# In the overflow tile of a routed MoE stage, rows are held on TensorE while w1 streams; a gate's split moves to GpSimd

## The chip, the cores and the metric

One core of a Trainium2 chip runs the whole program as one launch. The metric is the device time of one execution in microseconds; the number quoted for a kernel is the median of its runs. The engines named below are TensorE (PE, with its weight loads shown apart as PEld), VectorE (DVE), ScalarE (ACT), GpSimd (POOL) and SyncE (SP).

## What is computed

Sparse attention gives 3072 rows of 512 values. Two mixture-of-experts layers with eight experts each follow. In the first one a row with a positive skip score goes to the expert of its largest gate logit, in the second one each expert takes exactly 384 rows, given out greedily by logit. The first layer is what the change is about:

```python
def _moe_ref(x, w_skip, w_gate, w1, w2):
    do_compute = x @ w_skip > 0
    xc = x[do_compute]
    logits = xc @ w_gate
    e_idx = np.argmax(logits, axis=1)
    ...                                   # gate_w: softmax value of the chosen expert
    for e in range(E):
        mask = e_idx == e
        h = np.maximum(xc[mask] @ w1[e], 0.0)
        y[mask] = gate_w[mask, None] * (h @ w2[e])
    out[do_compute] = xc + y
```

Then `_moe2_ref` takes `logits = x @ w_gate` over the new rows (the "second gate"), sorts all of them, assigns rows under the cap of 384 for each expert, and computes `relu(x @ w1[e]) @ w2[e]`.

## The kernel before, in words

**Precision.** Every large product is made of three: each float32 operand is split into a rounded high part and the rest, the low part (`xh`, `xl`, `w1h`, `w1l`, `hh`, `hl`, `w2h`, `w2l`). ACT makes a high part, DVE subtracts it from the source to make the low part, and TensorE multiplies high by high, high by low and low by high.

**Stages.** Attention comes first. The first MoE layer then runs over blocks k = 0 to 7, one for each expert, with up to 224 rows (a tile of 128 and one of 96, `WIDE1` = 224). An expert with more than 224 rows leaves the rest to overflow tiles of 128 rows; block E (= 8) is the first of these. A count `n` made on the chip says how many there are, and with this data there is one: the path `n > 0` and `n < 2` runs, and the loop `more(k)` for further tiles does not. A search for the thresholds of the second layer's assignment follows, and then the second layer over its eight experts.

**A block.** For block k TensorE first makes h, turned (1024 hidden values along partitions, rows along columns): `h_products(k, s, m)`, m = 0 to 7, each twelve matmuls that hold a 128x128 piece of w1 and stream `WIDE1` = 224 columns of x, in block E too, where only 128 columns are real. Bank `ph[m % 4]` receives them. ACT (`one_block`, L1309) writes relu(h) as `hh`, DVE (L1399) makes `hl`. ACT (L1312) and DVE (L1402) also split the eight pieces of w2. `y_products(k, t, c)`, c = 0 to 7 (L1159), holds the 128 rows' hidden values of piece c and streams 512 columns of w2 three times. DVE's `y_keep` (L1420) scales by the gate and adds x, POOL's `scatter` (L1012) stores the rows.

**The second gate.** Between the h groups of block k, `z_part(k - 1, ...)` makes the second gate's logits of block k - 1: TensorE turns its finished rows (L1115), four transposes at a time, ACT copies them (L1298), TensorE multiplies by the gate (L1125 with three bf16 parts of the gate for blocks 0 to 6, L1133 in float32 for block 7 and the overflow tile), DVE copies the result to `zo` (L1391, L1393), and POOL scatters it to a table in HBM (L1021). In which group of block k a part comes is said by `z_at(k)`: `Z_AT` = (1, 3, 4, 7) in general, `Z_LAST` = (2, 3, 4, 5) for block E. The three bf16 parts of the gate, `wg2_parts`, are made by `split_gate2()` on DVE (L1501 to L1504), as the first thing of `count_extra()`, which stands in `y_keep` of block 0 between its two tiles.

**The end of the layer.** When both scatters of block 7's logits have landed, POOL raises `z_all`, SP loads the whole table back (L980, `logits`), and DVE takes its limits (L1589 to L1591) after the `y_keep` of the overflow tile. TensorE turns the limits (L1231), runs two filler matmuls (L1207, `keep_busy`), makes the overflow tile's own logits (L1133) and places them (L1252); DVE opens the search (from L1624).

Each engine runs its own instruction list in the order of the code and waits on semaphores. On ACT, `next_parts(E, ...)` has split w1 and x of the overflow tile before `one_block(E)` starts.

## Time and profile before

| what | us |
|---|---|
| median of 3 runs | 798.75 (798.06 to 798.95) |
| profiled execution | 799.55 |
| its span, first to last instruction | 797.8 |
| last y matmul of block 7 to first y matmul of the overflow tile | 434.61 to 447.95 |
| last y matmul of the overflow tile | 453.20 |
| search opens on DVE | 458.47 |

The profile is of one execution, with its own time; the median is of others, 0.8 us shorter. In a row of the order of time the first number is the start in us from the span's start and the second the duration; a bracket at the end gives the idle time before it on its engine and what ended it. Matmuls overlap, so their durations add up to more than the time that they take; the pace is the distance from start to start.

### The profile page before, as it was taken

How to read it: one execution, taken by the hardware profiler on the slowest of the kernel's cores; microseconds unless marked ns; L12 is line 12 of the kernel's file. 1: busy time of each engine (PE TensorE's matmuls, PEld its weight loads, DVE VectorE, ACT ScalarE, POOL GpSimd, SP SyncE). 2: the span in 40 equal slices, each digit the busy share in tenths (PEclk: the TensorE clock that was granted, in tenths of full speed). 3: DMA queues.
4: the chain of work that ended last, by engine and by line, in shares of the span. 5: the costliest groups of instructions: out<-in, count | busy, mean ns of one | idle time of the engine just before them, and what ended most of it. 6: DMA issues, size and time to landing. Idle time of an engine off the chain costs nothing. (4 is left out here: it accounts for less than half of the span.)

```text
span 797.8 us, 15936 instructions
## 1 busy us (share of the span) xinstructions
PE 746.6 (94%) x5652; PEld 669.1 (84%) x5652; DVE 549.1 (69%) x1509; ACT 460.7 (58%) x935; POOL 164.5 (21%) x185
## 2 busy tenths in 40 slices
PE   2899999999959999999999929999999999999997
PEld 2899999999939888899888826888888888888895
DVE  6878778778378979787767567767676757585420
ACT  3889889899536554565555305554545363636360
POOL 8100000000030232222222102141424232323221
PEclk9999999999969999999999959999999999999999
DMA  8999999986265576645663016767767676759851
GB/s 179 219 217 243 233 210 237 203 236 152 104 202 174 191 245 231 213 148 180 230 236 124 17 54 221 189 212 189 220 186 221 184 222 184 223 170 309 231 120 44
DMA packets 64107, 151.66 MB, mean 190 GB/s; under 512 B 12294, under 2 KB 15750, under 8 KB 64016
## 3 DMA queue, kind: packets, MB, share of 16 engines
q1 hardware_dynamic: 52512, 114.77, 49.0%
q0 software_dynamic: 11504, 35.72, 18.0%
q8 instruction: 52, 0.85, 0.5%
q14 instruction: 39, 0.32, 0.1%
HBM read 118.84 MB, written 16.67 MB: 170 GB/s over the span
## 5 line engine op out<-in xcount | busy, mean ns | idle before, releaser
L1912 PE MATMUL r_ph<-r_xh,r_w1h 128*128 128x384 f32 x256 | 90.6, 354 | 0.3 <-ACT r_xh L2026 0.3
L1912 PE MATMUL r_ph<-r_xh,r_w1l 128*128 128x384 f32 x256 | 86.2, 337 | 0.0
L1912 PE MATMUL r_ph<-r_xl,r_w1h 128*128 128x384 f32 x256 | 85.8, 335 | 0.0
L599 ACT ACTIVATE pr<-pr,nmx 128x232 f32<-128x232 f32 (+1 forms) x192 | 79.9, 467 | 4.9 <-DVE nmx L705 3.5
L1149 PE MATMUL m_ph<-m_xh,m_w1h 128*128 128x224 f32 x288 | 80.5, 279 | 0.1
L1149 PE MATMUL m_ph<-m_xh,m_w1l 128*128 128x224 f32 x288 | 79.0, 274 | 0.0
L1149 PE MATMUL m_ph<-m_xl,m_w1h 128*128 128x224 f32 x288 | 79.0, 274 | 0.0
L705 DVE CUSTOM_DVE_ANT_0 pr<-sc,bias 128x232 f32<-128x232 f32 (+1 forms) x192 | 65.0, 375 | 19.1 <-PE sc L473 17.6
L606 ACT ACTIVATE prt<-tp 128x384 f32<-128x384 f32 (+1 forms) x128 | 65.4, 536 | 21.5 <-PE tp L485 18.0
L1926 PE MATMUL r_py<-r_w2h,r_hh 128*128 128x512 f32 x192 | 76.3, 397 | 0.0
L1926 PE MATMUL r_py<-r_w2h,r_hl 128*128 128x512 f32 x192 | 75.1, 391 | 0.0
L1926 PE MATMUL r_py<-r_w2l,r_hh 128*128 128x512 f32 x192 | 74.9, 390 | 0.0
L472 PE MATMUL sc<-kk,qh 128*128 128x256 f32 x192 | 59.2, 329 | 14.9 <-POOL shut L438 14.2
L513 PE MATMUL op<-vo,prt 128*128 128x128 f32 x384 | 69.8, 277 | 3.0 <-ACT prt L606 3.0
L1309 ACT ACTIVATE m_hh<-m_ph 128x224 fp32r<-128x224 f32 (+1 forms) x72 | 25.2, 350 | 82.0 <-PE m_ph L1149 80.8
L2030 ACT ACTIVATE r_hh<-r_ph 128x384 fp32r<-128x384 f32 x64 | 31.2, 488 | 61.1 <-PE r_ph L1912 61.1
L516 PE MATMUL op<-vp,prt 104*128 104x128 f32 x320 | 62.3, 276 | 0.0
L2016 ACT ACTIVATE r_w1h<-r_w 128x1024 fp32r<-128x1024 f32 x32 | 33.6, 1059 | 45.2 <-DMA r_w<-moe_w 45.1
L513 PEld LDWEIGHTS op<-vo,prt 128*128 128x128 f32 x384 | 55.9, 192 | 3.7 <-ACT prt L606 2.2
L1149 PEld LDWEIGHTS m_ph<-m_xh,m_w1h 128*128 128x128 f32 x288 | 55.3, 192 | 1.0 <-ACT m_xh L1276 0.6
L1149 PEld LDWEIGHTS m_ph<-m_xl,m_w1h 128*128 128x128 f32 x288 | 55.3, 192 | 0.3
L1149 PEld LDWEIGHTS m_ph<-m_xh,m_w1l 128*128 128x128 f32 x288 | 55.3, 192 | 0.0
(327 smaller groups left out, 1970.1 us busy)
## 6 DMA issues: line engine op xcount, KB each, us to landing
r_w<-moe_w SPq DMA_DIRECT2D x64, 512.0 KB, 5.1
m_w<-moe_w SPq DMA_DIRECT2D x36, 512.0 KB, 4.8
row_buf<-moe_w SPq DMA_DIRECT2D x9, 2048.0 KB, 8.4
r_w2l<-r_w POOLq DMA_DIRECT2D x32, 512.0 KB, 5.3
k_raw<-kI SPq DMA_DIRECT2D x64, 208.0 KB, 7.0
q_raw<-qT SPq DMA_DIRECT2D x64, 192.0 KB, 7.5
vo<-vL SPq DMA_DIRECT2D x16, 384.0 KB
x_rows<-row_buf SPq DMA_DIRECT2D x4, 1536.0 KB, 6.3
```

The source lines that it names most:

```text
L472: nc.tensor.matmul(to, qh[s][:, hh, q], kk[s][:, hh, keys], start=True, stop=False)
L513: last = nc.tensor.matmul(o, w[:, t * P:(t + 1) * P], v_own(s, hh, i), start=True, stop=(i == 0))
L516: last = nc.tensor.matmul(o, w[0:CA, c * P:(c + 1) * P], v_band(s, hh, i - 1), start=False, stop=True)
L599: nc.scalar.activation(pr[n % PRS][:, t, lo:CW], pr[n % PRS][:, t, lo:CW], ACT.Exp, bias=nmx[n % PRS][:, t:t + 1], scale=-1.0).then_inc(ex ...
L606: nc.scalar.activation(prt[item % PRTS][:, 0:w], tp[item % 2][:, 0:w], ACT.Copy).then_inc(kept, 1)
L705: v.tensor_tensor_reduce(out=pr[n % PRS][:, t, lo:CW], in0=src, in1=bias0[:, h, :] if tile0 else bias[:, h, :], scale=-SCALE, scalar=3e38, ...
L1149: last = nc.tensor.matmul(ph[m % 4][:, 0:WIDE1], w[:, c, m * P:(m + 1) * P], x[s][:, c, 0:WIDE1], start=(c == 0 and a == 0), stop=(c == KC ...
L1309: nc.scalar.activation(hh[:, m, 0:W], ph[m % 4][:, 0:W], ACT.Relu).then_inc(h_high, 1)
L1912: last = nc.tensor.matmul(ph[m % 4][:, 0:CAP], w[:, c, m * P:(m + 1) * P], x[:, c, :], start=(c == 0 and a == 0), stop=(c == KC - 1 and a ...
L1926: last = nc.tensor.matmul(py[g % 2][:], h[:, c, t * P:(t + 1) * P], w[:, c, :], start=(c == 0 and a == 0), stop=(c == FC - 1 and a == 2))
L2016: nc.scalar.activation(w1h[:, c, :], w1[:, c, :], ACT.Copy).then_inc(w1_high, 1)
L2030: nc.scalar.activation(hh[:, m, :], ph[m % 4][:, 0:CAP], ACT.Relu).then_inc(h_high, 1)
```

## The change

1. **`one_tile(k)` takes the place of `one_block(k, ...)`** for block E and for further overflow tiles, on TensorE, ACT and DVE. TensorE's `hidden(k, half, chunks)` holds the 128 rows (`x[0][:, c, 0:P]`, high or low) and streams 512 columns of w1: 2 halves of 4 chunks of 3 matmuls, 24 matmuls of 512 columns in place of 96 of 224. h then lies with rows along partitions in `ph[0]` and `ph[1]`. ACT keeps relu(h) in `hidden_rows` (the storage of `xg[1]`), two operations of 512 columns (`keep_hidden`); TensorE turns it, eight transposes into `ph[2]` and `ph[3]` (`turn_hidden`); ACT copies each half into `hh` (`high_part`) and DVE makes `hl` (`low_part`), 512 columns each. `y_products` stays, with its waits counted in halves.
2. **Order inside the tile.** The parts of the second gate for block 7 stand after chunks 0 and 1, after chunks 2 and 3, and between the two `turn_hidden`. `Z_LAST` is gone. ACT now waits at the start of the tile until block 7's rows are kept (`y_kept`), since `xg[1]` is overwritten.
3. **`split_gate2()`** leaves DVE's `count_extra()`; its four operations stand at the end of POOL's list for the attention stage, behind a wait for the tables' loads.

The core of the diff:

```diff
@@ POOL, end of the attention stage
+                pool.wait_ge(loaded, TABLE_LOADS * 16)
+                keep_link(g.tensor_copy(wg2_parts[:, :, 0, :], wg2[:]))
+                keep_link(g.tensor_tensor(wg2_rest[:], wg2[:], wg2_parts[:, :, 0, :], ALU.subtract))
+                keep_link(g.tensor_copy(wg2_parts[:, :, 1, :], wg2_rest[:]))
+                keep_link(g.tensor_tensor(wg2_parts[:, :, 2, :], wg2_rest[:], wg2_parts[:, :, 1, :], ALU.subtract))
@@ TensorE
+                def hidden(k, half, chunks):
+                    for c in chunks:
+                        if half == 0:
+                            for part in (x_high, x_low, w1_high, w1_low):
+                                pe.wait_ge(part, KC * k + c + 1)
+                        for a, (x, w) in enumerate(((xh, w1h), (xl, w1h), (xh, w1l))):
+                            last = nc.tensor.matmul(ph[half][:], x[0][:, c, 0:P], w[:, c, half * 4 * P:(half + 1) * 4 * P],
+                                                    start=(c == 0 and a == 0), stop=(c == KC - 1 and a == 2))
+                    if c == KC - 1:
+                        last.then_inc(h_done, 1)
+
+                def turn_hidden(k, half):
+                    pe.wait_ge(rows_kept, 2 * (k - E) + half + 1)
+                    for m in range(4):
+                        last = nc.tensor.transpose(ph[2 + half][:, m * P:(m + 1) * P], hidden_rows[:, (4 * half + m) * P:(4 * half + m + 1) * P], ident[:])
+                    last.then_inc(rows_turned, 1)
...
+                def one_tile(k):
+                    hidden(k, 0, (0, 1))
+                        z_part(k - 1, 1, 0)
+                    hidden(k, 0, (2, 3))
+                        z_part(k - 1, 1, 1)
+                    hidden(k, 1, range(KC))
+                    turn_hidden(k, 0)
+                        z_part(k - 1, 1, 3)
+                    turn_hidden(k, 1)
+                    pe.wait_ge(y_kept, tiles_before(k))
+                    for c in range(FC):
+                        y_products(k, 0, c)
@@ DVE
                 def count_extra():
-                    split_gate2()
                     z_rows_of_slots()
```

How the instructions stand in TensorE's list of the overflow tile before, from the second gate's multiplication (`m_pt<-wg,m_yt`) of block 7 to the y products (`m_py`); `m_ph` is h, turned:

```order
L1149 MATMUL m_ph<-m_xl,m_w1h 128x224
L1149 MATMUL m_ph<-m_xh,m_w1l 128x224
L1133 MATMUL m_pt<-wg,m_yt 128x8 x4
L1133 MATMUL m_pt<-wg,m_yt 96x8 x4
L1149 MATMUL m_ph<-m_xh,m_w1h 128x224
...
L1159 MATMUL m_py<-m_w2h,m_hh 128x512
```

The same place in TensorE's list of the changed kernel (`m_ph<-ident,m_xg` turns the relu rows, which lie in `xg[1]`):

```order
L1203 MATMUL m_ph<-m_w1h,m_xh 128x512
L1203 MATMUL m_ph<-m_w1h,m_xl 128x512
L1203 MATMUL m_ph<-m_w1l,m_xh 128x512
L1211 MATMUL m_ph<-ident,m_xg 128x128 x4
L1144 MATMUL m_pt<-wg,m_yt 128x8 x4
L1144 MATMUL m_pt<-wg,m_yt 96x8 x4
L1211 MATMUL m_ph<-ident,m_xg 128x128 x4
L1172 MATMUL m_py<-m_w2h,m_hh 128x512
```

Two groups of h (24 matmuls) stood behind the gate's multiplication; now all of h stands ahead of it, and four transposes stand on each side.

ACT's list of the changed kernel for the whole overflow tile (`m_w2h` are the pieces of w2, `m_yt` the turned rows of block 7, `m_xg<-m_ph` the relu, `m_hh<-m_ph` the copy of the turned half):

```order
L1370 ACTIVATE m_w2h<-row_buf 128x512 x2
L1346 ACTIVATE m_yt<-m_pt 128x224 x2
L1370 ACTIVATE m_w2h<-row_buf 128x512
L1374 ACTIVATE m_xg<-m_ph 128x512
L1370 ACTIVATE m_w2h<-row_buf 128x512
L1346 ACTIVATE m_yt<-m_pt 128x224 x2
L1370 ACTIVATE m_w2h<-row_buf 128x512
L1374 ACTIVATE m_xg<-m_ph 128x512
L1378 ACTIVATE m_hh<-m_ph 128x4x128
L1370 ACTIVATE m_w2h<-row_buf 128x512
L1378 ACTIVATE m_hh<-m_ph 128x4x128
L1370 ACTIVATE m_w2h<-row_buf 128x512 x2
```

Before, this list was eight pairs of `m_hh` (128x128) and `m_w2h`, with the two pairs of `m_yt` behind the third and the fourth; now five pieces of w2 stand ahead of the first `m_hh`.

DVE's list of the changed kernel from the first w2 pieces of the overflow tile (`m_zo` is the copy of block 7's logits):

```order
L1493 TENSOR_TENSOR m_w2l<-row_buf,m_w2h 128x512 x5
L1497 TENSOR_TENSOR m_hl<-m_ph,m_hh 128x4x128
L1474 COPY m_zo<-m_pt 128x8
L1474 COPY m_zo<-m_pt 96x8
L1493 TENSOR_TENSOR m_w2l<-row_buf,m_w2h 128x512
L1497 TENSOR_TENSOR m_hl<-m_ph,m_hh 128x4x128
L1493 TENSOR_TENSOR m_w2l<-row_buf,m_w2h 128x512 x2
```

Before, `m_zo` stood behind the sixth piece of w2 and six `m_hl` of 128 columns; now it stands behind the first half's `m_hl`.

## Rows read from the trace of the kernel before

**Rows 1.** The page's row of h, high times high

```profile
L1149 PE MATMUL m_ph<-m_xh,m_w1h 128*128 128x224 f32 x288 | 80.5, 279 | 0.1
```

**Rows 2.** Waits of TensorE, 264 to 462 us: total us, times, longest

```profile
PE m_pt L1115 <- DVE row_buf L1420: 0.2, 1, 0.2
PE m_ph L1231 <- DVEq L1592: 0.2, 1, 0.2
```

**Rows 3.** Order of time, TensorE, overflow tile: start, duration, line, operation

```profile
434.84 0.27 PE L1149 MATMUL m_ph<-m_xh,m_w1h 128*128 128x224 f32 x1
...
438.85 0.56 PE L1115 MATMUL m_pt<-ident,row_buf 128*128 128x128 f32 x4
...
443.70 1.64 PE L1133 MATMUL m_pt<-wg,m_yt 128*128 128x8 f32 x16
...
447.95 0.40 PE L1159 MATMUL m_py<-m_w2h,m_hh 128*128 128x512 f32 x1
...
453.20 0.40 PE L1159 MATMUL m_py<-m_w2h,m_hl 128*128 128x512 f32 x1
```

**Rows 4.** Order of time, TensorE, four transposes of 128 rows

```profile
483.99 0.66 PE L1898 MATMUL r_ph<-ident,r_xg 128*128 128x128 f32 x4
484.48 0.38 PE L1934 MATMUL r_py<-lane_grid,onesb 128*128 128x512 bf16 x1
```

**Rows 5.** Order of time, ACT, then DVE, overflow tile

```profile
437.71 0.28 ACT L1309 ACTIVATE m_hh<-m_ph 128x128 fp32r<-128x128 f32 x1 [0.49 <-PE m_ph L1149]
437.89 0.63 ACT L1312 ACTIVATE m_w2h<-row_buf 128x512 fp32r<-128x512 f32 x1
...
435.04 0.75 DVE L1420 SCALAR_TENSOR_TENSOR row_buf<-m_py,gates,m_xg 96x512 f32<-96x512 f32 x1 [3.10 <-PE m_py L1159]
...
438.02 0.29 DVE L1399 SCALAR_TENSOR_TENSOR m_hl<-m_ph,m_hh 128x128 fp32r<-128x128 f32 x1
438.54 0.69 DVE L1402 TENSOR_TENSOR m_w2l<-row_buf,m_w2h 128x512 fp32r<-128x512 f32 x1 [0.23 <-ACT m_w2h L1312]
```

**Rows 6.** The page's row of ACT's larger h

```profile
L2030 ACT ACTIVATE r_hh<-r_ph 128x384 fp32r<-128x384 f32 x64 | 31.2, 488 | 61.1 <-PE r_ph L1912 61.1
```

**Rows 7.** Order of time and DMA issues, block 7's logits (KB, us to landing)

```profile
445.38 0.23 DVE L1393 COPY m_zo<-m_pt 128x8 f32<-128x8 f32 x2
...
450.43 0.34 SPq L980 DMA_DIRECT2D logits<-gate_logits  x1
...
logits<-gate_logits SPq DMA_DIRECT2D x1, 96.0 KB, 2.0
```

**Rows 8.** Order of time, all engines, end of the layer

```profile
453.75 0.75 DVE L1420 SCALAR_TENSOR_TENSOR row_buf<-m_py,gates,m_xg 128x512 f32<-128x512 f32 x1 [3.02 <-PE m_py L1159]
...
454.41 0.34 DVE L1589 TENSOR_REDUCE m_limits<-logits 128x1 f32<-128x192 f32 x1
...
455.98 0.95 PE L1133 MATMUL m_pt<-wg,m_yt 128*128 128x8 f32 x8
```

**Rows 9.** Order of time, DVE and TensorE, end of block 0

```profile
261.28 0.17 DVE L1501 CAST wg_parts<-wg 128x32 bf16<-128x32 f32 x1
...
262.16 0.17 DVE L1434 TENSOR_SCALAR m_lanes<-m_pt 128x16 f32<-128x16 f32 x1
```

**Rows 10.** The page's row of DVE's costliest operation in attention

```profile
L705 DVE CUSTOM_DVE_ANT_0 pr<-sc,bias 128x232 f32<-128x232 f32 (+1 forms) x192 | 65.0, 375 | 19.1 <-PE sc L473 17.6
```

**Rows 11.** Waits from 26 to 236 us; order of time, POOL

```profile
POOL m_never L1024 <- POOLq L214: 201.6, 1, 201.6
...
18.68 0.34 POOL L446 CAST ids<-idsf 128x48 bf16<-128x48 f32 x1
```

**Rows 12.** Busy us by stretch (PE, PEld, DVE, ACT, POOL), granted clock

```profile
445.00:450.00 5.00, 5.00 (x38) 4.66 (x37) 2.84 (x10) 1.59 (x4) 2.35 (x2) 1.00 0.01 1
...
460.00:462.00 2.00, 0.00 (x0) 0.00 (x0) 1.21 (x7) 0.00 (x0) 0.00 (x0) 0.71 0.00 0
478.00:480.00 2.00, 2.00 (x15) 1.12 (x14) 1.00 (x4) 0.81 (x1) 0.00 (x0) 0.50 0.84 307
```

More of the change, by code:

```diff
@@ L897, in z_at, with hidden_before @@
             def z_at(k):
-                return () if not isinstance(k, int) or k == 0 else Z_LAST if k == E else Z_AT
+                return Z_AT if k else ()
+            def hidden_before(k):
+                return FC * k if isinstance(k, int) and k <= E else 2 * k + (FC - 2) * E
             def in_parts(k):
@@ L1154, in y_products @@
                     if t == 0:
-                        for part in (h_high, h_low, w2_high, w2_low):
+                        for part in (h_high, h_low):
+                            pe.wait_ge(part, FC * k + c + 1 if isinstance(k, int) and k < E else hidden_before(k) + c // 4 + 1)
+                        for part in (w2_high, w2_low):
                             pe.wait_ge(part, FC * k + c + 1)
@@ L1314, in one_block, with one_tile, w2_part, keep_hidden @@
                             z_part(k - 1, z_at(k).index(m))
+                def one_tile(k):
+                    act.wait_ge(y_done, tiles_before(k))
+                    act.wait_ge(y_kept, tiles_before(k))
+                    act.wait_ge(w2_loaded, 16 * k + 16)
+                    def w2_part(m):
+                        nc.scalar.activation(w2h[:, m, :], w2[:, m, :], ACT.Copy).then_inc(w2_high, 1)
+                    def keep_hidden(half):
+                        act.wait_ge(h_done, hidden_before(k) + half + 1)
+                        nc.scalar.activation(hidden_rows[:, half * 4 * P:(half + 1) * 4 * P], ph[half][:], ACT.Relu).then_inc(rows_kept, 1)
+                    def high_part(half):
+                        act.wait_ge(rows_turned, 2 * (k - E) + half + 1)
+                        nc.scalar.activation(hh[:, 4 * half:4 * half + 4, 0:P], ph[2 + half][:].rearrange("p (m n) -> p m n", n=P), ACT.Copy).then_inc(h_high, 1)
+                    w2_part(0)
+                    w2_part(1)
+                    if isinstance(k, int):
+                        z_part(k - 1, 0)
+                    w2_part(2)
+                    keep_hidden(0)
+                    w2_part(3)
+                    if isinstance(k, int):
+                        z_part(k - 1, 1)
+                    w2_part(4)
+                    keep_hidden(1)
+                    high_part(0)
+                    w2_part(5)
+                    high_part(1)
+                    w2_part(6)
+                    w2_part(7)
                 for s in range(2):
@@ L1336, in _ @@
                     next_parts(E, 0, P)
-                    one_block(E, P)
+                    one_tile(E)
                     for i in range(4):
@@ L1406, in one_block, with one_tile, w2_part, low_part @@
                             gates_of_slots()
+                def one_tile(k):
+                    def w2_part(m):
+                        dve.wait_ge(w2_high, FC * k + m + 1)
+                        v.tensor_tensor(w2l[:, m, :], w2[:, m, :], w2h[:, m, :].bitcast(F32), ALU.subtract).then_inc(w2_low, 1)
+                    def low_part(half):
+                        dve.wait_ge(h_high, hidden_before(k) + half + 1)
+                        v.tensor_tensor(hl[:, 4 * half:4 * half + 4, 0:P], ph[2 + half][:].rearrange("p (m n) -> p m n", n=P),
+                                        hh[:, 4 * half:4 * half + 4, 0:P].bitcast(F32), ALU.subtract).then_inc(h_low, 1)
+                    for m in range(5):
+                        w2_part(m)
+                    low_part(0)
+                    if isinstance(k, int):
+                        z_part(k - 1, 1, 3)
+                    w2_part(5)
+                    low_part(1)
+                    w2_part(6)
+                    w2_part(7)
                 def y_keep(k, s):
@@ L1645, in more @@
                     next_parts(k, 0, P)
-                    one_block(k, P)
+                    one_tile(k)
                     y_keep(k, 0)
@@ L1653, in _ @@
                 with dve.If(n > 1):
-                    one_block(E, P)
+                    one_tile(E)
                     y_keep(E, 0)
```

22 lines of the change are left out of this document (11 added, 11 removed).

## The prediction, made before the changed kernel was run

> **What bounds the kernel now.** I read the page's costliest groups first. One row of h in the first MoE layer has 288 matmuls [rows 1], 32 for each of nine blocks: eight experts and one overflow tile. So the overflow tile runs, and its h streams 224 columns like every other block's. The view of who waited for whom for TensorE, from the end of block 0 to the end of the layer, has only two rows, of 0.2 us each [rows 2]. In these 200 us TensorE is the bound: what is taken from its list shortens the layer, as long as nobody makes it wait. The view in order of time gives the tile [rows 3]: h starts at 434.84, the y products at 447.95, the last of these at 453.20. ACT and DVE have idle time between their pieces there [rows 5]. The rows at the end of the layer show a second chain beside the y products: block 7's logits are scattered, loaded back, and DVE's limits need them [rows 7, 8].
>
> **TensorE's share of the tile.** The 36 matmuls of 224 columns from 434.84 to 438.85 [rows 3] have a pace of 4.01 / 36 = 0.111 us. Removed: 96 x 0.111 = 10.7 us. Added: 24 matmuls of 512 columns. The y products have this very shape, 128 held columns and 512 streamed in float32 parts, and their 24 take (453.20 - 447.95) / 23 = 0.228 us each [rows 3], so 5.5 us. Added too: eight transposes of 128 rows. Four of them take 484.48 - 483.99 = 0.49 us [rows 4], so 1.0 us. The block 7 parts (two groups of four transposes and the sixteen narrow matmuls) are in both kernels and only change place. Sum: -10.7 + 5.5 + 1.0 = **-4.2 us**, y products from about 443.7 in place of 447.95. The bounds of a transposing group are the 0.49 us and nothing at all (the weight loads might hide them): gain 4.2 to 5.2.
>
> **Does the new chain hold TensorE up?** New is that h passes ACT, TensorE, ACT and DVE before the first y product. By the paces above, 24 matmuls and the two transposing groups of block 7 end at 434.84 + 5.5 + 0.84 = 441.16. The 0.84 is what rows 3 leave from 434.84 to 443.70 beside 72 matmuls of 0.111. The last matmul is done some 0.2 us later. ACT's relu of 512 columns out of PSUM isn't in this tile. From 0.28 us for 128 columns [rows 5] and 0.49 for 384 [rows 6] a line gives 0.59; four times the small one is 1.12, the upper end. ACT also needs the first half's copy (0.59), and DVE its low part: 0.69 us for 512 columns out of SBUF [rows 5], upper end four times 0.29 = 1.16. With my values: 441.4 + 0.6 + 0.6 + 0.7 = 443.3. TensorE meanwhile turns the first half (0.49), does the sixteen narrow matmuls (from 443.70 to 447.95 less 24 x 0.111, so 1.58) and turns the second half (0.49): 443.7. The chain is hidden with **0.4 us** to spare, and I take no wait, since the line through two measured sizes is nearer than four separate operations. With all upper ends it ends at 444.8, and TensorE waits 1.1 us. The second half is needed only by the fifth y chunk, twelve matmuls or 2.7 us later, and is ready about 445.2 against 446.5. The w2 pieces cost ACT 0.63 and DVE 0.69 each [rows 5]; the last is ready near 446.3 against a need at 448.5. ACT's new wait for block 7's kept rows ends at 435.8 (DVE's operation from 435.04, 0.75 us) [rows 5]; it holds the w2 pieces behind it, the first of which came behind a relu before, and so not ahead of the first twelve matmuls (434.84 + 12 x 0.111 = 436.2). It costs nothing.
>
> **Where the gain can be caught: the logits.** DVE copies block 7's logits at 445.38, SP loads the table at 450.43, and it lands 2.0 us later, 452.43 [rows 7]. The limits start at 454.41, right behind the kept y rows [rows 8], so this chain has 2.0 us of slack now. In the changed order the narrow matmuls start at 441.16 + 0.49 = 441.65 in place of 443.70 [rows 3], **2.05 us** earlier, against 4.2 for the y rows. DVE is free for the copy at 443.3, as it is due. So the table lands at 450.4 while the y rows would allow the limits at 450.2: the slack is used up, and 0.2 us of the gain goes to a new wait for a DMA. TensorE turns the limits and runs two fillers ahead of the tile's own logits, from 455.98 [rows 8], so this wait is passed on in full. Gain so far **4.0 us**; if landing counts from the end of the issue (0.34 us, rows 7), 3.7.
>
> **The gate's split.** On DVE its four operations take from 261.28 to 262.16 [rows 9], 0.88 us, ahead of the keep of block 0's second tile, for which TensorE waits 0.2 us [rows 2]. All but these 0.2 us were hidden; gain **0.2 us**, bounds 0 and 0.25. On GpSimd they stand where it sits idle for 201.6 us [rows 11]; a cast of 48 columns takes 0.34 us there, so four such are 1.4 us, hidden by that idle time. Nothing else is behind the new wait on GpSimd's list until the MoE layer. For DVE the bounds are no delay, and 1.4 us in attention if it were shut out for all of it; I take none, since DVE's own work there leaves it idle for 19.1 us, of which 17.6 are waits for TensorE [rows 10].
> The Trainium skill has a rule against this part ("SBUF — State Buffer", section "Who interferes with whom"): a DVE instruction with two SBUF inputs and a GpSimd instruction that reads SBUF shut each other out, the later one waits for the whole of the earlier. No row here shows such a block; by the rule DVE could lose up to those 1.4 us once, and the sum would be 2.8 in place of 4.2 if TensorE passed all of it on.
>
> **Sum.** 4.0 + 0.2 = 4.2 us. The profiled execution took 799.55 us, its span 797.8: after, 795.3 and 793.6. The median of the runs is 0.8 below that execution, so the predicted median is 798.75 - 4.2 = **794.5 us**. The search and the second layer follow the limits through dependences alone, so I let them shift as they are.
>
> **Rivals.**
> 1. *The relu chain ends last.* With the upper ends above, y starts 1.1 us late, and DVE's copy of the logits, which stands behind the first low part, comes at 444.8 in place of 443.3, so the table lands at 451.9. Gain 454.4 - 451.9 + 0.2 = 2.7: 796.05 us. For it: four PSUM passes in a row where there was one pair. Against: the two ACT sizes lie on a flat line.
> 2. *The logits decide by more.* If GpSimd's scatters or the load take 1 us longer from their earlier start, the limits wait 1.2 us: 795.5. For it: their slack is exactly used up. Against: they start into a stretch with no other transfer.
> 3. *Slower: the clock falls in the tile.* TensorE's granted clock is 1.00 from 445 to 450, with the narrow matmuls in it, and 0.50 (1.2 GHz) from 478 to 480 after the search's short bursts; it fell between 460 and 462, a stretch with no TensorE work in it [rows 12]. If it fell when the turning starts at 441.2, the 2.6 us up to the y products and their 5.5 us would take twice as long: +8.1, 802.6 us. From 4.2 us of work at 1.2 GHz on, the change no longer pays. Against: the stretch has no idle time by my sum, and the narrow matmuls and transposes of the kernel before left the clock at 1.00. The Trainium skill speaks for this one ("TensorE: Matmul & The Clock Gate", section "Part 4: PE-mode transpose"): transposes don't count as work for the clock in the way that matmuls do. By it eight more transposes bring the fall nearer; the row from 445 to 450 is against it here.
> 4. *The gain is given back later.* The search and the fillers ahead of the second layer come 4.2 us earlier. From 478 to 480 the clock was still at 0.50 [rows 12]. If it rises later against the fillers, TensorE enters the second layer at 1.2 GHz. To eat all of the gain this needs 4.2 us of work there at the full clock's price done at half: 798.7, no change. Against: TensorE was busy for all of those 2 us, so it works towards the rise well ahead of the layer.
>
> That the change doesn't do what it says is out: the tile's matmuls are in the trace, and the order of instructions shows theirs replaced.
>
> **Chances.** Forecast (793.6 to 795.4) 0.66; rival 1 0.12; rival 2 0.13; rival 3 0.04; rival 4 0.05. What a measurement of this kernel can tell from no change is about 0.2%, 1.6 us: faster means under 797.15, where the forecast and rivals 1 and 2 lie, and half of rival 4's partial cases, 0.92. Within 0.2%: 0.05. Slower: 0.03, the full form of rival 3. The range takes in rivals 1 and 2 and the unknown costs. Below: transposing groups at no cost bring the narrow matmuls, and the table, another 0.49 us forward (gain 4.7, 794.05), less 0.45 us, half of the spread of the three runs. Above: rival 1 and about as much: **793.6 to 796.6**.
>
> **What would show it.** Right: 24 matmuls of 512 columns at 0.228 us; y products starting about 443.5 with no idle TensorE ahead of them; the wait of 0.2 us at the end of block 0 gone and what follows 0.2 us earlier; a DVE idle time of some tenths ahead of the limits, ended by the load; the table load issued about 448.2. Wrong: idle TensorE ahead of the first y product, ended by DVE (rival 1); a wait of over 1 us ahead of the limits (rival 2); a granted clock under 1.00 between 440 and 450 (rival 3); the opening of the search 4.2 us earlier but the end less so (rival 4).

## The result, and the profile after

The changed kernel takes **794.01 us** (median of four runs, 793.26 to 794.20), beside 798.64 (also of four) for the kernel before. The ratio is 0.9936, 95% interval 0.9924 to 0.9949. Applied to the 798.75 us of the first table, that is a gain of 5.1 us, 4.1 to 6.1, or about 793.6 us; the two medians by themselves differ by 4.6 us. The prediction had a gain of 4.2 and a range from 793.6 up. The time by the ratio lies at that very edge, too near to call it inside or outside, and the interval of the gain holds the forecast. The prediction was right in sign and in the tile's mechanism; its gain was too small, and the bounds of one of its terms were wrong.

The profiled execution took 794.11 us with a span of 792.4 (before: 799.55 and 797.8), so 5.4 us less between first and last instruction. The mean granted clock was 0.975 in both.

TensorE in the overflow tile, in order of time, of the changed kernel (start, duration, line, operation, the idle time ahead of it and what ended it). It answers to [rows 3]:

```profile
434.15 0.39 PE L1203 MATMUL m_ph<-m_w1h,m_xh 128*128 128x512 f32 x1
...
438.88 0.39 PE L1203 MATMUL m_ph<-m_w1l,m_xh 128*128 128x512 f32 x1
...
440.24 0.39 PE L1203 MATMUL m_ph<-m_w1l,m_xh 128*128 128x512 f32 x1
440.47 0.60 PE L1211 MATMUL m_ph<-ident,m_xg 128*128 128x128 f32 x4
440.91 1.64 PE L1144 MATMUL m_pt<-wg,m_yt 128*128 128x8 f32 x16
442.40 0.64 PE L1211 MATMUL m_ph<-ident,m_xg 128*128 128x128 f32 x4
442.79 0.48 PE L1172 MATMUL m_py<-m_w2h,m_hh 128*128 128x512 f32 x1
...
448.12 0.40 PE L1172 MATMUL m_py<-m_w2h,m_hl 128*128 128x512 f32 x1
```

From 434.15 to the first y product are 8.64 us; before, from 434.84 to 447.95, 13.11. No row of TensorE's matmuls or weight loads there has idle time in a bracket, and the starts follow one another at the usual pace: the relu chain doesn't hold TensorE up. The seven matmuls from 438.88 to 440.24 lie 0.227 us apart, the pace that the y products had. The first turning group costs 440.91 - 440.47 = 0.44 us, the second 442.79 - 442.40 = 0.39.

ACT and DVE beside it, the relu chain and the copy of block 7's logits; it answers to [rows 5, 7]:

```profile
440.67 0.60 ACT L1374 ACTIVATE m_xg<-m_ph 128x512 f32<-128x512 f32 x1 [1.02 <-PE m_ph L1203]
441.16 0.59 ACT L1378 ACTIVATE m_hh<-m_ph 128x512 fp32r<-128x512 f32 x1
441.79 0.69 DVE L1497 TENSOR_TENSOR m_hl<-m_ph,m_hh 128x512 fp32r<-128x512 f32 x1 [1.41 <-ACT m_hh L1378]
442.58 0.23 DVE L1474 COPY m_zo<-m_pt 128x8 f32<-128x8 f32 x2
```

The row at 441.79 ends at 442.48, and the first y product starts at 442.79: 0.3 us between them. Not all of it is slack, as e5_relu_in_four_pieces shows below.

The end of the layer, all engines, in order of time; it answers to [rows 7, 8]:

```profile
443.68 0.99 POOL L1032 DMA_INDIRECT gate_logits<-m_zo,m_zrows  x1 [6.33 <-DVE m_zo L1474]
444.98 1.41 POOL L1032 DMA_INDIRECT gate_logits<-m_zo,m_zrows  x1 [0.30 <-issue]
447.66 0.34 SPq L991 DMA_DIRECT2D logits<-gate_logits  x1
448.65 0.75 DVE L1522 SCALAR_TENSOR_TENSOR row_buf<-m_py,gates,m_xg 128x512 f32<-128x512 f32 x1 [1.94 <-PE m_py L1172]
449.63 0.35 DVE L1683 TENSOR_REDUCE m_limits<-logits 128x1 f32<-128x192 f32 x1 [0.23 <-DMA logits<-gate_logits]
```

The limits now wait 0.23 us for the loaded table, right behind the kept rows. From start to start it costs a little more: they start 0.98 us behind the keep at 448.65, where in the kernel before it was 454.41 - 453.75 = 0.66 [rows 8], so 0.3 us.

Where the gain lies. The columns are distances between marks in order of time in each kernel's trace, in us. Block 0 runs from ACT's first `hh` to the turning of block 0's rows on TensorE; the tile from DVE's keep of block 7's last rows to the limits; the entry from the search's `best` (L1624 before) to the first `r_hh` of the second layer; the second layer from there to the end of the span.

| kernel | block 0 | blocks 1 to 7 | tile | entry | second layer |
|---|---|---|---|---|---|
| before | 25.88 | 167.77 | 19.37 | 33.44 | 305.90 |
| before, again | 25.88 | 167.87 | 19.37 | 33.04 | 305.98 |
| changed | 25.50 | 167.85 | 15.28 | 33.15 | 305.52 |
| changed, again | 25.48 | 167.85 | 15.28 | 32.90 | 305.52 |
| tile alone | 25.89 | 167.77 | 15.20 | 33.21 | 305.76 |
| split alone | 25.49 | 167.86 | 19.37 | 32.92 | 305.45 |

Before against changed: tile -4.09, block 0 -0.38, blocks 1 to 7 +0.08, entry -0.29, second layer -0.38. The rest of the 5.4 us, -0.39, lies ahead of block 0's first `hh`, 241.39 us from the span's start before and 241.00 changed. Five runs whose kernels are the same up to the tile (changed, again, e4, e5 and e9 below) reach this mark anywhere from 240.56 to 241.58, so I read nothing into it. The entry too differs by 0.2 to 0.4 between two executions of one kernel.

The second layer's column needs a cut of its own. From the last y product to the end of the span the two executions of the kernel before take 5.50 and 5.75 us, so the end of the program scatters by 0.25. From the first `r_hh` to the last y product they take 300.40 and 300.23, the changed kernel 300.06 and 300.03: about 0.2 to 0.4 us are gained on TensorE itself.

### The profile page after: what moved, and what is told of

Same layout as the page of the kernel before. It is cut to its first block and busy times, and to the rows that moved or that the text cites. A ratio compares the mean times of both kernels' runs of the same rounds, so it can differ in the third digit from the quotient of the medians.

```text
span 792.4 us, 15792 instructions
## 1 busy us (share of the span) xinstructions
PE 740.9 (94%) x5585; PEld 662.7 (84%) x5588; DVE 548.1 (69%) x1499; ACT 461.7 (58%) x931; POOL 165.9 (21%) x189
## 5 line engine op out<-in xcount | busy, mean ns | idle before, releaser
L1160 PE MATMUL m_ph<-m_xh,m_w1h 128*128 128x224 f32 x256 | 71.5, 279 | 0.1
L1160 PE MATMUL m_ph<-m_xl,m_w1h 128*128 128x224 f32 x256 | 70.2, 274 | 0.0
L1160 PE MATMUL m_ph<-m_xh,m_w1l 128*128 128x224 f32 x256 | 70.2, 274 | 0.0
L1357 ACT ACTIVATE m_hh<-m_ph 128x224 fp32r<-128x224 f32 x64 | 22.9, 358 | 69.0 <-PE m_ph L1160 69.0
L1172 PE MATMUL m_py<-m_w2h,m_hh 128*128 128x512 f32 (+1 forms) x136 | 55.3, 407 | 0.0
L490 PE MATMUL tp<-ident,pr 128*128 128x128 f32 x352 | 54.4, 273 | 0.2 <-ACT prt L611 0.2
L1172 PE MATMUL m_py<-m_w2l,m_hh 128*128 128x512 f32 (+1 forms) x136 | 53.3, 392 | 0.0
```

Of the source, the lines that this page charges most:

```text
L490: last = nc.tensor.transpose(tp[item % 2][:, c * P:(c + 1) * P], parts[c], ident[:])
L1160: last = nc.tensor.matmul(ph[m % 4][:, 0:WIDE1], w[:, c, m * P:(m + 1) * P], x[s][:, c, 0:WIDE1], start=(c == 0 and a == 0), stop=(c == KC ...
L1172: last = nc.tensor.matmul(py[t % 2][0:r, :], h[:, c, t * P:t * P + r], w[:, c, :], start=(c == 0 and a == 0), stop=(c == FC - 1 and a == 2))
```

## The experiments

**Theory.** The gain is the tile's 24 wide matmuls in place of 96 narrow ones, less two turning groups, with the table load catching 0.2 us; the split gives the stall at the end of block 0. **Rivals.** The gain of the tile comes from its 96 dead columns; the relu chain or the load is close to deciding; the clock can fall in this tile; and for the part that I had not foreseen, that VectorE's list, not the tile, changed the second layer.

### The two kernels again

> The kernel before, unchanged, as a second profile of it. The 5.4 us between the two profiled spans fall into 0.34 up to the MoE layer's first w1 parts, 0.35 at the end of block 0, 4.1 from there to the limits, 0.3 at the entry of the second layer and 0.35 within it. Theory (the first, fourth and fifth come from one execution, not from the kernel): this profile differs from the first one of the same kernel by some tenths of a us in these three stretches, either way, and the ratio to the kernel before is 1.000 within 0.001. Rival (the change shortens them too): they are within 0.1 us of the first profile.

The kernel before again: 799.12 us, ratio 0.9994 (0.9985 to 1.0003).

> The changed kernel as it is, timed in five rounds. My sum of 4.2 us gives a ratio of 0.9947; the tile and the split as the profile shows them, 4.1 + 0.35 = 4.45 us, give 0.9944; all of the 5.4 us of the two profiled spans would be 0.9932. Theory: 0.994 to 0.995. Rival (something outside the tile and block 0 gained another 0.9 us): 0.9932 or less.

The changed kernel again: 793.83 us, ratio 0.9937 (0.9924 to 0.9950). Both repeat, in time and in the table above: the marks of tile and block 0 to within 0.02 us. Of the stretches outside them the entry moved by some tenths between two executions, as e0's theory said, and the second layer didn't (0.08 us): its shortening isn't chance of one execution. e1's 0.9937 lies between its theory (0.994 to 0.995) and its rival (0.9932), and the interval holds both.

### One part at a time

> The tile's part alone: the gate is split on VectorE again, as before. Theory: the wait of TensorE at the end of block 0 is back at 0.2 to 0.35 us, first limits operation of the layer 4.1 us earlier than before relative to the tile's start; gain 4.0 to 4.1 us, ratio 0.9949. Rival (the split is worth more than its wait, since GpSimd's list or VectorE's backlog in block 1 matters): the gain falls to 3.5 us or less, ratio over 0.9955.

```diff
@@ the changed kernel, POOL
-                keep_link(g.tensor_copy(wg2_parts[:, :, 0, :], wg2[:]))
... (the wait and the other three operations too)
@@ DVE
                 def count_extra():
+                    split_gate2()
                     z_rows_of_slots()
```

Measured: 794.85 us, ratio 0.9955 (0.9941 to 0.9968), 3.6 us, between the theory's 4.0 and the rival's 3.5, and the interval holds both. The trace decides for the tile: 15.20, so 4.17 shorter, with block 0 at 25.89 as in the kernel before.

> The gate's split alone: four operations on GpSimd in attention, the tile as before. Theory: gain 0.2 to 0.35 us, ratio 0.9996 to 0.9998, which the times can hardly tell from none; in the trace TensorE's wait ahead of the transposes of block 0's rows is gone and block 1 is 0.2 to 0.35 us earlier relative to block 0's first h. Rival (GpSimd and VectorE shut each other out in attention): a VectorE operation with two SBUF inputs is longer than its 0.94 or 1.02 us beside the four operations, and attention ends up to 1 us later. The Trainium skill ("SBUF — State Buffer", "Who interferes with whom") would have the later one of the two wait.

```diff
@@ the kernel before, POOL, end of the attention stage
+                pool.wait_ge(loaded, TABLE_LOADS * 16)
+                keep_link(g.tensor_copy(wg2_parts[:, :, 0, :], wg2[:]))
+                ...
@@ DVE
                 def count_extra():
-                    split_gate2()
                     z_rows_of_slots()
```

Measured: 798.07 us, ratio 0.9987 (0.9979 to 0.9996), so 1.0 us, 0.3 to 1.7. Tile 19.37 as before, block 0 25.49, second layer 305.45. The two parts add up: 3.6 + 1.0 = 4.6, beside 5.1 measured together, within the intervals. All of the block 0 gain is the split's and all of the tile's gain the tile's. The split is worth more than the 0.2 us that I gave it: the trace shows 0.39 at block 0 alone.

Why block 0 gives 0.39 where the view of waits says 0.2. TensorE there, in order of time, of the kernel before:

```profile
266.75 0.27 PE L1149 MATMUL m_ph<-m_xh,m_w1l 128*128 128x224 f32 x1
267.27 0.61 PE L1115 MATMUL m_pt<-ident,row_buf 128*128 128x128 f32 x4 [0.25 <-DVE row_buf L1420]
```

and of the split alone:

```profile
266.56 0.28 PE L1154 MATMUL m_ph<-m_xh,m_w1l 128*128 128x224 f32 x1
266.67 0.55 PE L1120 MATMUL m_pt<-ident,row_buf 128*128 128x128 f32 x4
```

The idle time in the bracket is counted from the end of the last matmul, 267.02, and that end lies 0.27 us behind its start though the next one may start 0.11 behind it. From start to start the stall is 267.27 - 266.75 - 0.11 = 0.41 us, and with the split gone the distance is the plain pace of 0.11. The row of the weight load at the same place shows nearly all of it:

```profile
267.27 0.40 PEld L1115 LDWEIGHTS m_pt<-ident,row_buf 128*128 128x128 f32 x4 [0.43 <-DVE row_buf L1420]
```

The first three of GpSimd's four operations of the changed kernel, and DVE's operation beside the first, in order of time:

```profile
69.59 1.02 DVE L686 TENSOR_TENSOR kk<-k_raw,kk 64x832 fp32r<-64x832 f32 x1 [0.94 <-ACT kk L598]
```

```profile
69.77 0.91 POOL L455 CAST wg_parts<-wg 128x32 bf16<-128x32 f32 x1 [47.63 <-DMA step_t<-steps]
70.77 0.25 POOL L456 TENSOR_TENSOR wg_rest<-wg,wg_parts 128x32 f32<-128x32 f32 x1
71.08 0.21 POOL L457 CAST wg_parts<-wg_rest 128x32 bf16<-128x32 f32 x1
...
```

The first cast took 0.91 us and a cast of the same shape two rows on 0.21. The first began 0.18 us into DVE's operation with two SBUF inputs and ended just behind it (70.68 against 70.61); DVE's 1.02 us is what this operation takes elsewhere. That is the case of the Trainium skill ("SBUF — State Buffer", section "Who interferes with whom"), with the later one, here GpSimd, waiting for the earlier. It isn't that the first cast is slow behind a long idle time: in the changed kernel's second execution the first cast took 0.21 us and the second operation, which began 0.26 us into DVE's, 0.90; in the split alone none of the four met such an operation of DVE, and all took 0.21 to 0.25. Where DVE's operation began just behind a GpSimd cast it lost a little itself: 1.05 us in that second execution, 1.08 in e8. In the changed kernel's profile it lost nothing.

### The logits earlier, and the second turning between y chunks

> In the overflow tile block 7's logits come earlier: TensorE turns the first half of the relu rows and makes the logits after half of the second h half, turns the second half behind the first y chunk; ACT's and VectorE's lists follow. The same instructions in number. Theory (the table load now ends last ahead of the limits, by some 0.2 us): the logits' copy is 1.3 us earlier relative to the tile's start, the table load is issued about 1.3 us earlier, VectorE's wait for it ahead of the limits is gone, y products still without a wait, search opens 0.2 to 0.3 us earlier than in the changed kernel; ratio to before 0.9940 to 0.9945. Rival (the chain of relu rows ends last): TensorE waits ahead of the fifth y chunk or the first, and nothing is gained or some tenths are lost.

```diff
@@ TensorE, one_tile
-                    hidden(k, 1, range(KC))
+                    hidden(k, 1, (0, 1))
                     turn_hidden(k, 0)
                     if isinstance(k, int):
                         z_part(k - 1, 1, 3)
-                    turn_hidden(k, 1)
+                    hidden(k, 1, (2, 3))
                     pe.wait_ge(y_kept, tiles_before(k))
                     for c in range(FC):
                         y_products(k, 0, c)
+                        if c == 0:
+                            turn_hidden(k, 1)
```

ACT's and DVE's lists follow it: the first half's copy ahead of the fifth piece of w2, the second relu behind the sixth. Measured: 794.34 us, ratio 0.9939 (0.9926 to 0.9952), tile 15.28: nothing gained. The limits follow the kept rows without a wait, so the load's part was as I read it; but this is TensorE then, in order of time, with ACT's second relu:

```profile
443.18 0.60 ACT L1376 ACTIVATE m_xg<-m_ph 128x512 f32<-128x512 f32 x1 [1.32 <-PE m_ph L1203]
...
443.44 0.40 PE L1172 MATMUL m_py<-m_w2h,m_hl 128*128 128x512 f32 x1
...
443.83 0.66 PE L1211 MATMUL m_ph<-ident,m_xg 128*128 128x128 f32 x4
...
450.10 0.34 DVE L1686 TENSOR_REDUCE m_limits<-logits 128x1 f32<-128x192 f32 x1
```

The turning starts 0.39 us behind the last y product of chunk 0 where the pace is 0.23: it waits for the relu, which ends at 443.78. These 0.16 us are lost under the modelled end of a matmul, so the matmul's row has no bracket; the weight load beside it has one, of 0.42 us, ended by ACT's `m_xg`. With them and some more about the restart the keep of the tile's rows comes 0.30 us later than in the changed kernel, which takes the place of the 0.3 that the load had cost. So the first half of the theory held, and the rival named what was then in the way.

> The tile of e4_logits_earlier (block 7's narrow matmuls in the middle of the second half of h), with the second turning moved behind the second y chunk. Everything is computed. If the 0.16 us of wait ahead of that turning and what it cost to go on again are what ate the 0.2 us of the vanished wait for the table: no wait ahead of it, the limits 15.0 to 15.1 us after the keep of block 7's last rows in place of 15.28, 793.7 to 793.9 in all. If turning between y chunks costs more than turning ahead of them (the weight loads of a y chunk are not prepared behind a transpose): 15.3 or more, no gain over the changed kernel.

```diff
@@ the kernel of e4_logits_earlier
-                        if c == 0:
+                        if c == 1:
                             turn_hidden(k, 1)
```

Measured: 794.89 us, ratio 0.9941 (0.9926 to 0.9957), tile 15.40. The first expectation fell. The wait ahead of the turning is gone, but the one for the low part of the same half has come. TensorE and DVE, in order of time:

```profile
444.39 0.60 PE L1211 MATMUL m_ph<-ident,m_xg 128*128 128x128 f32 x4
444.75 0.48 PE L1172 MATMUL m_py<-m_w2h,m_hh 128*128 128x512 f32 x1
...
445.66 0.69 DVE L1499 TENSOR_TENSOR m_hl<-m_ph,m_hh 128x512 fp32r<-128x512 f32 x1 [0.61 <-ACT m_hh L1380]
...
445.99 0.40 PE L1172 MATMUL m_py<-m_w2h,m_hl 128*128 128x512 f32 x1
...
446.45 0.48 PE L1172 MATMUL m_py<-m_w2h,m_hh 128*128 128x512 f32 x1
```

The fifth chunk starts 0.46 us behind its forerunner, 0.23 late, and 0.1 behind the end of the low part (446.35). The time came out as its rival said (15.3 or more), but not for the rival's reason, that turning between y chunks costs more by itself: the turning took 444.75 - 444.39 = 0.36 us, less than in the changed kernel. None of the three orders beats another by more than 0.12 us; the tile is within some tenths of having every side chain end at the same time.

### The relu chain made longer

> The changed kernel with the relu, its copy and the low part done in four operations of 128 columns each instead of one of 512, in both halves. It prices rival 1 of the prediction: ends of 4 x 0.28 and 4 x 0.29 us. Theory: the chain gets 3 x 0.2 to 3 x 0.5 us longer (operations overlap by about 0.1 us each), VectorE's low part of the first half ends 0.5 to 1.4 us later, against 0.3 us of cover: TensorE waits 0.3 to 1.1 us ahead of the first y product, and the limits come 0.5 to 1.3 us later than in the changed kernel, since the logits' copy stands behind the low part. Rival (the chain has more cover than it seems, as TensorE's first y product is held by something else): no wait and the same time.

```diff
@@ the changed kernel, ACT (the copy to hh and DVE's low part likewise)
-                        nc.scalar.activation(hidden_rows[:, half * 4 * P:(half + 1) * 4 * P], ph[half][:], ACT.Relu).then_inc(rows_kept, 1)
+                        for m in range(4):
+                            last = nc.scalar.activation(hidden_rows[:, (half * 4 + m) * P:(half * 4 + m + 1) * P], ph[half][:, m * P:(m + 1) * P], ACT.Relu)
+                        last.then_inc(rows_kept, 1)
```

Measured: 793.99 us, ratio 0.9943 (0.9930 to 0.9956), the tile 15.64 in place of 15.28. ACT, DVE and TensorE, in order of time:

```profile
440.08 0.79 ACT L1375 ACTIVATE m_xg<-m_ph 128x128 f32<-128x128 f32 x4 [0.84 <-PE m_ph L1203]
...
440.73 0.82 ACT L1381 ACTIVATE m_hh<-m_ph 128x128 fp32r<-128x128 f32 x4
...
441.58 0.88 DVE L1502 TENSOR_TENSOR m_hl<-m_ph,m_hh 128x128 fp32r<-128x128 f32 x4 [1.62 <-ACT m_hh L1381]
...
442.67 0.47 PE L1172 MATMUL m_py<-m_w2h,m_hh 128*128 128x512 f32 x1 [0.23 <-issue]
```

Against the keep of block 7, DVE's low part ends 0.57 us later and the y products start 0.47 us later (8.91 for 8.44), the limits 0.36. So of the 0.3 us between the low part's end and the first y product only 0.1 was slack: even when TensorE waited, it started 0.21 us behind that end. The chain was hidden in the changed kernel, and it bounds the tile as soon as it grows by more than a tenth. Four operations of 128 columns take 0.79 us together, not the 4 x 0.28 that my rival 1 added up: behind one another they overlap.

### The dead columns, or the number of matmuls

> The kernel before, with w1 held as before, but the overflow tile streams only its 128 real columns in place of 224 in its 96 matmuls of h. No instruction added. Theory (what the tile pays for is the number of weight loads as much as the columns: a load of 128x128 takes 0.19 us in the rows): the pace falls from 0.111 to 0.06 to 0.10 us, and 96 of them gain 1 to 5 us; by columns alone it would be 0.111 x 128 / 224 = 0.063, gain 4.6 us, as much as the change itself. Rival (the weight load sets the pace already): 0.111 stays and nothing is gained. The Trainium skill ("TensorE: Matmul & The Clock Gate", Part 2) gives about 0.081 us for such pairs with 128 columns, which would be 2.9 us.

```diff
@@ the kernel before, TensorE, h_products
-                            last = nc.tensor.matmul(ph[m % 4][:, 0:WIDE1], w[:, c, m * P:(m + 1) * P], x[s][:, c, 0:WIDE1],
+                            W = width(k)
+                            last = nc.tensor.matmul(ph[m % 4][:, 0:W], w[:, c, m * P:(m + 1) * P], x[s][:, c, 0:W],
```

`width(k)` is 128 for the overflow tile: the old tile without its 96 dead columns. Measured: 801.75 us, ratio 1.0037 (1.0025 to 1.0049), **slower**. TensorE and its weight loads at the tile's start, and TensorE near its end, in order of time:

```profile
434.83 0.28 PE L1150 MATMUL m_ph<-m_xh,m_w1h 128*128 128x128 f32 x1
...
435.95 0.27 PE L1150 MATMUL m_ph<-m_xl,m_w1h 128*128 128x128 f32 x1
...
446.34 0.41 PE L1150 MATMUL m_ph<-m_xl,m_w1h 128*128 128x128 f32 x1
446.55 0.41 PE L1150 MATMUL m_ph<-m_xh,m_w1l 128*128 128x128 f32 x1
...
448.58 0.63 PE L1160 MATMUL m_py<-m_w2l,m_hh 128*128 128x512 f32 x1
449.01 0.63 PE L1160 MATMUL m_py<-m_w2h,m_hl 128*128 128x512 f32 x1
```

```profile
434.88 0.19 PEld L1150 LDWEIGHTS m_ph<-m_xl,m_w1h 128*128 128x128 f32 x1
```

Ten distances from 434.83 to 435.95 give 0.112 us a matmul, the same as with 224 columns. The theory's 0.06 to 0.10 and the page's 0.081 didn't come; the rival, that 0.111 stays, did. So the columns beyond 128 cost nothing in this stream: each matmul has a load of 128x128 held values, 0.19 us by its row and overlapping its neighbours, one for every 0.11 us (that it is the load that sets it is the nearest reading; no run changed the load alone). Here cutting columns from 224 to 128 saves nothing and cutting the number of matmuls does; the tile's gain is the second.

The other half of the result, which no expectation had, is the clock. The view by stretch (PE, PEld, DVE, ACT and POOL busy, then the granted clock, DMA share, GB/s):

```profile
...
446.00:447.00 1.00, 1.00 (x9) 1.00 (x8) 0.37 (x2) 0.80 (x2) 0.80 (x1) 0.67 0.00 0
447.00:453.00 6.00, 6.00 (x18) 4.94 (x18) 2.51 (x8) 0.80 (x2) 1.31 (x1) 0.50 0.07 18
453.00:454.00 1.00, 1.00 (x6) 0.82 (x5) 0.00 (x0) 0.00 (x0) 0.00 (x0) 0.92 0.00 0
```

From 446.3 to about 453 the granted clock is 0.50 (1.2 GHz), with TensorE shown busy all the time, and the y products stand 0.43 us apart. The tile is 22.54 us long in place of 19.37, 3.2 more. The clock was 1.00 from 434 to 446 us, the whole stream of 128-column matmuls, and the fall came behind it. Before the change, the same count of matmuls with 224 columns, and the same narrow gate matmuls, kept 1.00 from 434 to 455. So the fall that I had as rival 3 exists in this very place; the change stays clear of it. The changed kernel by stretch:

```profile
440.00:445.00 5.00, 5.00 (x37) 4.47 (x36) 3.20 (x8) 3.24 (x6) 1.01 (x2) 1.00 0.00 0
445.00:450.00 5.00, 4.94 (x25) 3.61 (x24) 2.68 (x8) 0.12 (x1) 1.39 (x1) 1.00 0.08 21
```

### The second layer's unexpected tenths

In the kernel before TensorE waits twice in the second layer for `r_upto` of DVE, in both of its executions. From the view of who waited for whom for TensorE, 480 us to the end:

```profile
PE r_pb L1879 <- DVE r_upto L2177: 0.5, 2, 0.3
```

Neither the changed kernel nor the split alone has this wait; the tile alone has one of 0.3. Behind one of the two, DVE in order of time in the kernel before has an idle time that the same rows of the changed kernel lack:

```profile
582.50 0.08 DVE L2122 DVE_READ_ACCUMULATOR2_ANT top<- 128x1 f32 x1
582.82 0.18 DVE L2138 TENSOR_TENSOR r_cmpb<-bestm,top 128x24 bf16<-128x24 f32 x1 [0.23 <-DVE top L2122]
```

```profile
577.39 0.08 DVE L2216 DVE_READ_ACCUMULATOR2_ANT top<- 128x1 f32 x1
577.51 0.18 DVE L2232 TENSOR_TENSOR r_cmpb<-bestm,top 128x24 bf16<-128x24 f32 x1
```

Nothing in these rows was changed; what differs is how many operations stand ahead in DVE's list. Three kernels tested this. All compute everything; the additions write tensors that nobody reads.

> The changed kernel, with four operations added on VectorE where the split stood before (first in count_extra): the same four shapes on the same gate, into tensors that nobody reads. GpSimd still makes the real split. Everything is computed as before. Theory A (the gain of the split is only a matter of how many operations stand in VectorE's list, there and behind it): block 0 gives 25.9 us from its first h to the turning of its rows (0.4 back), the second layer's waits for r_upto return, and from the first r_hh to the end are 305.8 to 306.1 us in place of 305.4 to 305.7; 794.3 to 794.6 in all. Theory B (GpSimd or the place of wg_parts' writer matters for the second layer): block 0 loses its 0.4 us again, the second layer stays at 305.4 to 305.7; 794.1 to 794.3.

> The changed kernel, with the same four operations into tensors that nobody reads, but earlier in VectorE's list, right behind the gates by tile and ahead of the first block's own operations. Everything is computed as before. Theory A (the second layer depends on where VectorE's instructions stand in its list): block 0 stays at 25.5 us, since nothing stands ahead of its kept rows, and the second layer goes back to 305.8 to 306.1 us; 794.2 to 794.5 in all. Theory B (it depends on GpSimd's part or on the time at which the tile's end falls): both stay as in the changed kernel, 25.5 and 305.4 to 305.7 us; 793.8 to 794.1.

> The changed kernel with ten operations more on VectorE, ahead of the first block's own, into tensors that nobody reads (e8_four_more_elsewhere had four); everything is computed as before. With four, VectorE's extra idle 0.2 us of the round at 577 to 582 us stood behind DVE_READ_ACCUMULATOR2 of r_which (L2257), and TensorE waited 0.3 us for r_upto. Theory A (the idle time belongs to a place counted in VectorE's list, so what stands ahead moves it): it now stands about six rows further up in the same round, around the reduction of r_cnt and the operations behind it, and in no other place of that round; TensorE's wait for r_upto stays, the last r_hh to the end part 305.5 to 305.9 us; 794.1 to 794.6 in all. Theory B (it belongs to the round's data or to the time): it stays behind r_which, or is gone.

```diff
@@ the changed kernel, DVE: at the head of count_extra (e7), or behind gates_by_tile (e8; e10 has ten such)
+                    link(v.tensor_copy(spare_parts[:, :, 0, :], wg2[:]))
+                    link(v.tensor_tensor(spare_rest[:], wg2[:], spare_parts[:, :, 0, :], ALU.subtract))
+                    link(v.tensor_copy(spare_parts[:, :, 1, :], spare_rest[:]))
+                    link(v.tensor_tensor(spare_parts[:, :, 2, :], spare_rest[:], spare_parts[:, :, 1, :], ALU.subtract))
```

| kernel | us | ratio (interval) | block 0 | wait for `r_upto` | second layer |
|---|---|---|---|---|---|
| e7, four in front of block 0's second keep | 794.23 | 0.9934 (0.9918 to 0.9951) | 25.88 | one, 0.3 | 305.54 |
| e8, four earlier | 794.16 | 0.9932 (0.9917 to 0.9947) | 25.48 | one, 0.3 | 305.58 |
| e10, ten earlier | 793.66 | 0.9937 (0.9920 to 0.9953) | 25.46 | none | 305.54 |

Block 0 is settled: four operations in front of the keep bring its stall back in full (25.88, and TensorE's row has the 0.25 again), the same four elsewhere don't. It is DVE's position that counts, not who makes `wg2_parts`.

The second layer is not. With four operations more the idle time on DVE came back, in another place of the same round; this is e8, in order of time:

```profile
580.72 0.08 DVE L2257 DVE_READ_ACCUMULATOR2_ANT r_which<- 128x1 f32 x1
581.07 0.15 DVE L2274 TENSOR_SCALAR expert<-r_which 128x1 int32<-128x1 f32 x1 [0.26 <-DVE r_which L2257]
```

So what stands ahead in the list does decide whether and where this 0.2 us appears: shown for four. But with ten it was gone, and not six rows further up as theory A asked; and the length of the second layer stayed at 305.54 to 305.58 with and without the wait, as theory B of e7 and e8 had it. The thirteen profiles, one execution each, fall in two groups. With the split on DVE (before, again, tile alone, e6) the second layer takes 305.76 to 306.09 us, with the split on GpSimd (the nine others) 305.42 to 305.74. By these whole lengths the groups all but touch, since the end of the program scatters; up to the last y product they are 300.23 to 300.40 and 299.90 to 300.11, 0.12 apart. The waits alone don't explain that division, and four and ten operations more didn't move a kernel across it. So the shortening goes with the split's place, by some 0.2 to 0.4 us, and through what it comes stays open, and so does the law of the idle time's place.

The added operations moved one thing more: blocks 1 to 7 take 167.55 to 167.60 us in e7, e8 and e10, where the changed kernel takes 167.85, some 0.05 less for nearly each block. No view of waits shows why.

## Why the prediction was right in its mechanism, and which step of it failed

- **The tile's sum** held within 0.25 us: y products 4.47 us earlier against the keep of block 7's last rows, where I had 4.23. The paces carried it (0.111 removed, 0.228 added). The term that was mis-sized is the turning group: 0.49 us from the second layer [rows 4], 0.44 and 0.39 here. The row that I took had a bf16 matmul of 512 columns behind it, other neighbours than the tile's. Two groups: 0.15 us. The narrow matmuls took 442.40 - 440.91 = 1.49 where I had 1.58: 0.09. Together that is the 0.24.
- **The relu chain** was sized to the hundredth (0.60, 0.59, 0.69), and hidden, but with less to spare than my 0.4: 0.3 us by the rows, and 0.1 by what e5 cost. My sum had no time between DVE's end and TensorE's start. Rival 1 was not the case. Its price was too high, though: with every pass in four pieces the y products were 0.47 us late, not 1.1, since operations of one engine overlap.
- **The logits** caught the limits for 0.23 us by the bracket and 0.3 from start to start, predicted 0.2; against the keep of block 7's last rows SP's load came 2.08 us earlier, predicted 2.05. The tile's gain at the limits was 4.09, predicted 4.03, since a part of what the turning gave was taken by this wait. e4 and e9 show that lifting it uncovers the second half's relu and then its low part, and rival 2, a further 1 us of it, wasn't the case.
- **The gate's split is the step that failed.** I gave it "gain 0.2 us, bounds 0 and 0.25", out of the idle time in the view of waits. It is 0.38 to 0.41 at block 0, because that idle time begins at a modelled end, and alone it measured 1.0 us (0.3 to 1.7), with a second layer 0.45 to 0.53 us shorter than in the two runs of the kernel before, 0.24 to 0.41 of it ahead of the last y product. That effect had no term at all, since I let everything behind the limits "shift as they are"; what carries it the runs don't show. The bounds were wrong, not only the value, and the range's low end rested on them: 4.7 + 0.45 us of gain.
- **The sum.** 4.09 + 0.38 - 0.08 at the limits and block 0 is 4.4, 0.2 over the forecast; 0.38 in the second layer makes 4.8. The interval of the ratio, 4.1 to 6.1, holds this and, at its edge, the forecast itself. The 5.1 in its middle has some tenths more, as has the span (5.4); the parts of the span that hold them, attention and the entry, moved as much between executions of the same instructions. That the time came so near the range's edge is thus in part the run's scatter, and in part the split. The half of the three runs' spread that I took for noise was too little for a range's edge.
- **Rival 3** had the right mechanism for another kernel: at 128 columns in each of the 96 matmuls the clock fell, at 512 in each of 24 it didn't. Of the two things that I held against it, no idle time isn't one: e6 had none either.
- **Rival 4** didn't come: the second layer was shorter, not longer.
- **GpSimd and DVE**: the block came, and hit mostly the engine that had time. Of the 1.4 us that the rule could have cost DVE at most 0.06 was seen (e8).

## What to carry to other kernels

Count matmuls, not columns, where each holds a fresh 128x128 float32 block: hold the operand that lets the stream be 512 wide, even at the price of turning the result, if the turning's chain fits under work that TensorE has anyway. Read a stall of TensorE from start to start against the pace of its neighbours; the idle time shown ahead of a matmul's row can be short by 0.16 us, and can be missing, where the weight load's row showed 0.43 and 0.42. When the last chain of a stretch is shortened, list the next ones with their slack: here three of them lay within some 0.3 us, and each reordering only changed which one was seen.

## What the runs showed of the hardware

- TensorE's pace with a new held block for each matmul was 0.111 to 0.112 us for 128 and for 224 float32 columns, and 0.228 for 512. The Trainium skill ("TensorE: Matmul & The Clock Gate", section "Part 2: What happens when you issue a matmul") gives 81 ns for 128 and 131 ns for 512 columns of such pairs; the measured paces here, of float32 operands, are longer, and they decide.
- The granted clock fell to 0.50 (e6, from 446.3 us) in a stretch where the profile shows TensorE busy all the time, behind 96 matmuls of 128 columns; behind 96 of 224 columns at the same pace it stayed at 1.00.
- DVE has an idle time of 0.2 us (0.23 before, 0.26 in e8) whose place in the program changed when four operations were added far ahead of it; with ten it was gone. TensorE's wait for it was 0.3 us, but the second layer's length didn't follow.
- A GpSimd cast of 32 columns took 0.91 us against 0.21 when it began inside a DVE operation with two SBUF inputs; DVE's own time did not change. DVE took 1.05 and 1.08 for 1.02 where it began just behind a GpSimd cast.
